# The fourth pair's weights asked for before the last token stores, and a pair's split in two

## The reference, cut to what matters

```python
# local attention: chunks of 32 queries, keys 16 left, 8 right, and 8 memory keys
out[:, :, c_start:c_end] = softmax(scale * q_c @ k_full.T) @ v_full

# Fourier mixing and first MLP
mixed = np.real(fft(fft(x, axis=1), axis=2))
u = x + mixed
un = (u - mu) / np.sqrt(var + 1e-06)
x = u + np.maximum(un @ w_ch1, 0.0) @ w_ch2          # 512 -> 2048 -> 512

# gated convolution
h = np.maximum(x @ w_in, 0.0)                        # 512 -> 1024
gate = 1.0 / (1.0 + np.exp(-conv3_over_tokens(h)))
y = (h * gate) @ w_out
```

## Time and profile before

| | us |
|---|---|
| median of three runs | 993.39 |
| lowest, highest | 991.74, 995.04 |
| profiled execution | 991.06 |
| its span in the trace | 989.3 |

### The profile page before, as it was taken

The page is one execution under the profiler, slowest core; times in us unless marked ns, Lnnn a source line. Parts: engine busy times, 40 slices in busy tenths (PEclk is TensorE's granted clock), DMA queues, the critical chain, the costliest instruction groups (busy, mean ns, idle before and its releaser), DMA issues.

```text
span 989.3 us, 15359 instructions
## 1 busy us (share of the span) xinstructions
PE 943.7 (95%) x6168; PEld 850.1 (86%) x6168; DVE 624.9 (63%) x1034; ACT 346.7 (35%) x583; POOL 221.1 (22%) x231
## 2 busy tenths in 40 slices
PE   5899997859999999999999999999999999999998
PEld 4788786858897998989989889898898898998997
DVE  5467759658586773776827767266486295393590
ACT  2444555314244231332312323124253254253341
POOL 5757758114020000000000000000024033042041
PEclk9999999889999999999999999999999999999999
DMA  9956733567435672544824536355120300301001
GB/s 336 356 178 235 277 120 108 217 230 283 184 142 231 215 260 67 195 147 155 308 79 161 181 117 233 129 160 179 60 70 1 128 1 22 106 0 42 22 1 64
DMA packets 50033, 148.41 MB, mean 150 GB/s; under 512 B 7856, under 2 KB 12080, under 8 KB 45616
## 3 DMA queue, kind: packets, MB, share of 16 engines
q1 hardware_dynamic: 44640, 85.16, 25.0%
q0 software_dynamic: 5184, 62.27, 16.8%
q10 hardware_dynamic: 144, 0.07, 0.0%
HBM read 115.50 MB, written 31.98 MB: 149 GB/s over the span
## 4 chain that ended last, share of the span: by engine, by line
PE 85%; DVE 5%; DMA 4%; POOL 3%; issue 1%; SPq 1%; ACT 1%; DVEq 0%; POOLq 0%; ACTq 0%
PE ps L995 25%; PE ps L975 22%; PE ps L1327 13%; PE ps L1337 13%; PE ps L543 5%; DMA k_win<-in_k 2%; PE ps L507 2%; DMA w_raw<-in_moe_w 1%; PE ps L1310 1%; PE ps L534 1%; PE ps L936 1%; DVE h_raw L890 1%; DVE w L813 1%; PE ps L517 1%; DVE h L894 1%
## 5 line engine op out<-in xcount | busy, mean ns | idle before, releaser
L995 PE MATMUL ps<-w,h 128*128 128x512 f32 x1152 | 267.3, 391 | 0.4 <-DVE h_raw L890 0.4
L995 PEld LDWEIGHTS ps<-w,h 128*128 128x128 f32 x1152 | 215.0, 188 | 44.6 <-DVE h_raw L890 0.8
L975 PE MATMUL ps<-x_hi,w 128*128 128x384 f32 x896 | 232.8, 338 | 11.5 <-DVE w L813 10.1
L975 PEld LDWEIGHTS ps<-x_hi,w 128*128 128x128 f32 x896 | 164.2, 190 | 12.8 <-DVE w L813 10.7
L890 DVE TENSOR_TENSOR h_raw<-h_raw,ps 128x384 f32<-128x384 f32 x224 | 122.8, 552 | 59.6 <-PE ps L975 53.5
L975 PE MATMUL ps<-x_lo,w 128*128 128x384 f32 x448 | 151.1, 337 | 0.0
L1327 PE MATMUL ps<-y_hi,v 128*128 128x384 f32 x512 | 130.6, 334 | 0.0
L806 ACT ACTIVATE h<-h_raw 128x384 fp32r<-128x384 f32 x128 | 67.0, 526 | 157.0 <-DVE h_raw L890 154.9
L1337 PE MATMUL ps<-v,g_hi 128*128 128x512 f32 x384 | 118.9, 391 | 0.0
L1395 POOL TENSOR_TENSOR g_lo<-conv,g_hi 128x768 fp32r<-128x768 f32 x32 | 68.8, 2154 | 185.7 <-ACT g_hi L1258 185.7
L1289 DVE SCALAR_TENSOR_TENSOR conv<-h_pad,taps,conv 128x768 f32<-128x768 f32 x64 | 100.5, 1570 | 2.3
(11 more groups left out here) (110 smaller groups left out, 1166.8 us busy)
## 6 DMA issues: line engine op xcount, KB each, us to landing
w<-w_scratch POOLq DMA_DIRECT2D x24, 1792.0 KB, 7.6
w_raw<-in_moe_w SPq DMA_DIRECT2D x80, 256.0 KB, 2.9
w_scratch<-w POOLq DMA_DIRECT2D x8, 1792.0 KB, 8.2
v_win<-in_v SPq DMA_DIRECT2D x48, 260.0 KB, 5.0
k_win<-in_k SPq DMA_DIRECT2D x48, 256.0 KB, 5.0
q_sb<-in_q SPq DMA_DIRECT2D x24, 256.0 KB, 4.6
y_scratch<-u SPq DMA_DIRECT2D x8, 768.0 KB, 4.6
y_in<-y_scratch SPq DMA_DIRECT2D x4, 1536.0 KB, 7.1
```

Of the source, the lines that this page charges most:

```text
L975: last = nc.tensor.matmul(result(n, i), a, b, start=(k == 0), stop=(k == 5))
L995: last = nc.tensor.matmul(ps[:, t, :], h[:, m, part, cols], w2[j % R2][:, weight], start=(m == 0 and i == 0), stop=(m == GROUP - 1 and i = ...
```

## The change

SP asks for pair 3's weights right after the stores of batch 2's tokens, ahead of the stores of batch 3's; that load no longer waits for the end of seq (only pair 2's does). POOL stores pair 0's weights ahead of the sums of pair 2, in mlp2. The tiles are renumbered so that the four sums and the three blocks each lie together, and a pair's split on ACT and DVE is two steps: `blocks1` on the three plain blocks (768 elements), which ACT does as soon as the load has landed, and `sums1` on the four sums (1024 elements) after POOL. DVE's `blocks1` also waits for the sums to be made. PE and the store wait for both. In `rest`, ACT does `blocks1` of pair n + 1 ahead of `keep_first(n)` and `sums1` behind it. `ORDER` has new places: in batch 3's end the new steps mlp14 to mlp16 (ACT) and mlp20 to mlp22 (DVE), `bl3.5` ahead of mlp10, `cm3.1` ahead of pair 2's split, which now stands among `mk3`; in batches 0 to 2 steps trade places with their neighbours; the tensor lines left out below are only wrapped anew. The core of the diff:

```diff
--- before.py
+++ after.py
...
-        "turn1.3 seq0.6 scores1.4 seq0.7 scores1.5 values1.1 dim0.1 turn1.4 values1.2 mix0.0 turn1.5 mix0.1 "
-        "values1.3 mix0.2 scores2.0 mix0.3 values1.4 mix0.4 mix0.5 scores2.1 turn2.0 values1.5 seq1.0 "
-        "scores2.2 seq1.1 turn2.1 seq1.2 turn2.2 seq1.3 scores2.3 seq1.4 values2.0 seq1.5 turn2.3 scores2.4 "
...
+        "turn1.3 seq0.6 scores1.4 seq0.7 values1.1 scores1.5 dim0.1 turn1.4 values1.2 mix0.0 turn1.5 mix0.1 "
+        "values1.3 mix0.2 scores2.0 mix0.3 values1.4 mix0.4 mix0.5 scores2.1 turn2.0 values1.5 seq1.0 turn2.1 "
+        "scores2.2 seq1.1 scores2.3 seq1.2 turn2.2 seq1.3 values2.0 seq1.4 turn2.3 seq1.5 scores2.4 values2.1 "
...
     "scalar": (
...
-        "split0.2 exp0.5 keep0.5 split0.3 exp1.0 bh0.0 split0.4 keep1.0 bh0.1 split0.5 bh0.2 exp1.1 bh0.3 "
-        "exp1.2 keep1.1 bh0.4 bh0.5 keep1.2 exp1.3 qs0.0 split1.0 bh0.6 mirror0.0 bh0.7 exp1.4 keep1.3 exp1.5 "
-        "qs0.1 keep1.4 mirror0.1 split1.1 keep1.5 split1.2 exp2.0 keep2.0 split1.3 exp2.1 bh1.0 split1.4 "
-        "bh1.1 keep2.1 exp2.2 bh1.2 split1.5 bh1.3 bh1.4 exp2.3 keep2.2 bh1.5 keep2.3 exp2.4 split2.0 qs1.0 "
+        "split0.2 exp0.5 keep0.5 split0.3 exp1.0 bh0.0 keep1.0 split0.4 bh0.1 split0.5 bh0.2 exp1.1 bh0.3 "
+        "exp1.2 keep1.1 bh0.4 bh0.5 keep1.2 exp1.3 qs0.0 split1.0 bh0.6 mirror0.0 bh0.7 exp1.4 keep1.3 qs0.1 "
+        "exp1.5 keep1.4 split1.1 mirror0.1 keep1.5 split1.2 exp2.0 split1.3 keep2.0 exp2.1 bh1.0 keep2.1 "
+        "split1.4 bh1.1 exp2.2 split1.5 bh1.2 exp2.3 bh1.3 keep2.2 bh1.4 bh1.5 split2.0 keep2.3 exp2.4 qs1.0 "
...
-        "qs2.1 split3.3 mirror2.1 split3.4 mlp1 bh3.0 split3.5 bh3.1 mlp2 mlp3 bh3.2 mlp7 bh3.3 bh3.4 mlp4 "
-        "bh3.5 mlp5 mlp8 mlp6 qs3.0 bh3.6 mirror3.0 bh3.7 mlp10 mlp9 qs3.1 mlp11 mirror3.1 mlp12 mlp13 "
+        "qs2.1 split3.3 mirror2.1 split3.4 mlp1 mlp14 bh3.0 split3.5 bh3.1 mlp2 mlp3 bh3.2 mlp7 bh3.3 bh3.4 "
+        "mlp4 bh3.5 mlp5 mlp15 mlp8 mlp6 qs3.0 bh3.6 mirror3.0 bh3.7 mlp16 mlp10 qs3.1 mlp9 mlp11 mirror3.1 "
+        "mlp12 mlp13 "
...
     "vector": (
...
-        "shift1.4 bl0.6 bl0.7 shift1.5 norm1.1 cm0.1 norm1.2 mk0.0 mk0.1 norm1.3 mk0.2 shift2.0 mk0.3 norm1.4 "
-        "mk0.4 shift2.1 mk0.5 norm1.5 bl1.0 shift2.2 bl1.1 mlp0 bl1.2 mlp1 bl1.3 shift2.3 mlp2 bl1.4 norm2.0 "
-        "bl1.5 shift2.4 norm2.1 cm1.0 bl1.6 shift2.5 bl1.7 norm2.2 shift3.0 cm1.1 norm2.3 mk1.0 mk1.1 norm2.4 "
-        "mk1.2 shift3.1 mk1.3 norm2.5 mk1.4 shift3.2 mk1.5 bl2.0 norm3.0 bl2.1 bl2.2 shift3.3 bl2.3 shift3.4 "
+        "shift1.4 bl0.6 bl0.7 norm1.1 shift1.5 cm0.1 norm1.2 mk0.0 mk0.1 norm1.3 mk0.2 shift2.0 norm1.4 mk0.3 "
+        "shift2.1 norm1.5 mk0.4 bl1.0 mk0.5 shift2.2 mlp0 bl1.1 shift2.3 bl1.2 mlp1 norm2.0 bl1.3 mlp2 bl1.4 "
+        "bl1.5 shift2.4 norm2.1 cm1.0 shift2.5 bl1.6 bl1.7 norm2.2 shift3.0 cm1.1 norm2.3 mk1.0 mk1.1 norm2.4 "
+        "mk1.2 shift3.1 mk1.3 norm2.5 mk1.4 shift3.2 mk1.5 norm3.0 bl2.0 bl2.1 bl2.2 shift3.3 bl2.3 shift3.4 "
...
-        "norm3.5 mk2.2 mk2.3 mlp6 mk2.4 mlp5 mk2.5 bl3.0 mlp9 bl3.1 mlp7 bl3.2 mlp8 bl3.3 mlp13 bl3.4 mlp10 "
-        "bl3.5 mlp11 mlp14 mlp12 cm3.0 bl3.6 bl3.7 mlp16 mlp15 cm3.1 mlp17 mk3.0 mk3.1 mk3.2 mk3.3 mlp18 "
-        "mk3.4 mlp19 mk3.5 "
+        "norm3.5 mk2.2 mk2.3 mlp6 mk2.4 mlp5 mk2.5 bl3.0 mlp9 bl3.1 mlp7 bl3.2 mlp8 bl3.3 mlp20 bl3.4 mlp13 "
+        "bl3.5 mlp11 mlp21 mlp10 cm3.0 mlp12 bl3.6 mlp14 bl3.7 mlp16 cm3.1 mlp17 mk3.0 mlp22 mk3.1 mlp15 "
+        "mk3.2 mk3.3 mlp18 mk3.4 mlp19 mk3.5 "
...
     "gpsimd": (
-        "tabs0.0 fold0.0 fold0.1 lower0.0 tabd0.0 fold0.2 lower0.1 fold0.3 lower0.2 fold0.4 lower0.3 fold0.5 "
-        "lower0.4 lower0.5 fold1.0 lower1.0 fold1.1 fold1.2 lower1.1 fold1.3 lower1.2 fold1.4 lower1.3 "
-        "fold1.5 lower1.4 lower1.5 fold2.0 fold2.1 lower2.0 lower2.1 fold2.2 fold2.3 lower2.2 fold2.4 "
+        "tabs0.0 fold0.0 fold0.1 lower0.0 tabd0.0 lower0.1 fold0.2 fold0.3 lower0.2 fold0.4 lower0.3 fold0.5 "
+        "lower0.4 lower0.5 fold1.0 lower1.0 fold1.1 lower1.1 fold1.2 fold1.3 lower1.2 fold1.4 lower1.3 "
+        "fold1.5 lower1.4 lower1.5 fold2.0 lower2.0 fold2.1 lower2.1 fold2.2 fold2.3 lower2.2 fold2.4 "
...
+            mlp_sync(sp, FOLDS)
             for i in range(FOLDS):
...
-    A11, S2, S1, S3, A12, S4, A22 = range(7)
+    S4, S3, S2, S1, A22, A11, A12 = range(7)
+    SUMS, BLOCKS = slice(S4, S1 + 1), slice(A22, A12 + 1)
...
-    w1_hi_ready, w1_ready = sem("w1_hi_ready"), sem("w1_ready")
+    a1_hi_ready, a1_ready, s1_hi_ready, s1_ready = (sem(f"{name}_ready") for name in ("a1_hi", "a1", "s1_hi", "s1"))
...
-        sp.dma_start(w1_raw[n % 3][:, A11:A12 + 1:A12 - A11, 1], w[2 * n][:, 0].rearrange("p (k c) -> p k c", k=2)
+        sp.dma_start(w1_raw[n % 3][:, A11:A12 + 1, 1], w[2 * n][:, 0].rearrange("p (k c) -> p k c", k=2)
...
-        sp.dma_start(w1_raw[n % 3][:, S1:A22 + 1:A22 - S1, 1], w[2 * n + 1][:, 0].rearrange("p (k c) -> p k c", k=2)
+        sp.dma_start(w1_raw[n % 3][:, S1:A22 + 1, 1], w[2 * n + 1][:, 0].rearrange("p (k c) -> p k c", k=2)
...
     def load_raw2(sp, j):
...
     def store_w1(pool, n):
-        pool.wait_ge(w1_ready, n + 1)
+        pool.wait_ge(a1_ready, n + 1)
+        pool.wait_ge(s1_ready, n + 1)
...
     def stream_w1(pool, n):
...
-        else:
+        elif i == 2:
...
     def on_scalar(act):
-        def weights1(n):
+        def blocks1(n):
+            act.wait_ge(ld_raw1[n % 3], 32 * (n // 3 + 1))
+            nc.scalar.activation(w1[n % 3][:, BLOCKS, 0], w1_raw[n % 3][:, BLOCKS, 1], ACT.Copy).then_inc(a1_hi_ready, 1)
...
+        def sums1(n):
...
-            nc.scalar.activation(w1[n % 3][:, :, 0], w1_raw[n % 3][:, :, 1], ACT.Copy).then_inc(w1_hi_ready, 1)
+            nc.scalar.activation(w1[n % 3][:, SUMS, 0], w1_raw[n % 3][:, SUMS, 1], ACT.Copy).then_inc(s1_hi_ready, 1)
...
         def weights2(j):
...
     def on_vector(dve):
-        def weights1(n):
-            dve.wait_ge(w1_hi_ready, n + 1)
-            nc.vector.tensor_tensor(w1[n % 3][:, :, 1], w1_raw[n % 3][:, :, 1], raw(w1[n % 3][:, :, 0]), ALU.subtract
-                                    ).then_inc(w1_ready, 1)
+        def lower1(n, part, ready):
+            nc.vector.tensor_tensor(w1[n % 3][:, part, 1], w1_raw[n % 3][:, part, 1], raw(w1[n % 3][:, part, 0]),
+                                    ALU.subtract).then_inc(ready, 1)
...
+        def blocks1(n):
...
+            dve.wait_ge(a1_hi_ready, n + 1)
+            dve.wait_ge(s_ready, n + 1)
+            lower1(n, BLOCKS, a1_ready)
...
+        def sums1(n):
+            dve.wait_ge(s1_hi_ready, n + 1)
+            lower1(n, SUMS, s1_ready)
...
         def weights2(j):
...
-        return (weights1, weights2, stats, variance, inverse_root, normalise, lower, lower_sums, combine, complete,
+        return (blocks1, sums1, weights2, stats, variance, inverse_root, normalise, lower, lower_sums, combine, complete,
...
     def on_tensor(pe):
...
-                pe.wait_ge(w1_ready, n + 1)
+                pe.wait_ge(a1_ready, n + 1)
+                pe.wait_ge(s1_ready, n + 1)
...
     def first_gpsimd(pool, k):
+        if k == 2:
+            store_w1(pool, 0)
...
     def first_scalar(act, k):
...
         elif k < 7:
...
         elif k < 10:
-            weights1(k - 7)
+            sums1(k - 7)
+        elif k > 13:
+            blocks1(k - 14)
...
     def first_vector(dve, k):
-        (weights1, weights2, stats, variance, inverse_root, normalise, lower, lower_sums, combine, complete,
+        (blocks1, sums1, weights2, stats, variance, inverse_root, normalise, lower, lower_sums, combine, complete,
...
         elif k < 16:
-            weights1(k - 13)
+            sums1(k - 13)
+        elif k > 19:
+            blocks1(k - 20)
...
-                    if n + 3 < PAIRS:
+                    if 0 < n < PAIRS - 3:
...
         def _(pool):
...
-            for n in range(PAIRS):
+            for n in range(1, PAIRS):
...
                 if n >= 2 and n + 1 < PAIRS:
...
         def _(act):
...
                     if n >= 2:
+                        early = 3 <= n + 1 < PAIRS and n + 1 not in (5, 6)
+                        if early:
+                            blocks1(n + 1)
...
-                        if 3 <= n + 1 < PAIRS and n + 1 not in (5, 6):
-                            weights1(n + 1)
+                        if early:
+                            sums1(n + 1)
...
                     if g == 0 and m in (0, 3):
-                        weights1(5 + m // 3)
+                        blocks1(5 + m // 3)
+                        sums1(5 + m // 3)
...
         def _(dve):
-            (weights1, weights2, stats, variance, inverse_root, normalise, lower, lower_sums, combine, complete,
+            (blocks1, sums1, weights2, stats, variance, inverse_root, normalise, lower, lower_sums, combine, complete,
...
                     if n >= 2:
+                        early = 3 <= n + 1 < PAIRS and n + 1 not in (5, 6)
...
```

(20 more changed lines are left out.)

## The result

| | before | changed |
|---|---|---|
| median of ten runs, us | 993.62 | 985.4 |
| lowest, highest | 991.74, 995.04 | 981.68, 990.54 |
| profiled execution | 991.06 | 982.31 |

The ratio is 0.9921, 95% interval 0.9901 to 0.9941: 7.8 us faster, 5.9 to 9.8 (the two medians differ by 8.2). The changed kernel's runs lie 9 us apart, those of before 3; on the chip of the first four experiments 24 runs of the kernel before lie 7.8 us apart (988.6 to 996.4), so a wide spread is not the changed kernel's alone.

What follows compares the result with a forecast made beforehand. PE, busy 95% of the span, was bounded by idle and half-clock stretches, chiefly 9.1 us waiting for pair 3's weights. Contraction 11.3 us earlier less 1.5 for the clock gave 9.8 us: 983.5 us forecast, range 979.0 to 988.5.

Steps and rivals of the forecast that it cites:

- L + 8.9: First contraction goes on 8.9 us after L, the landing of pair 4's load; L forecast 213.8, contraction 222.7.
- the 1.5 us that were to be paid for the clock: First contraction: PE idles 4.2 us, the clock then falls and costs 1.5 us of the gain.
- Part 1: Split in two, at dim3.0: starts at 169.5; an extra DVE instruction costs 0.3 us; mlp4 ends about 1.3 us earlier.
- Part 2: mix3.0 starts 3.5 us earlier after 1.2 us idle; full clock saves 1.5 us; pair 2 starts at 200.1.
- Part 3: Early load of pair 3: goes out at 187.3, lands by 194; pair 3 starts at 208.9, 12.9 us earlier.
- What is late next: After pair 3's start, pair 4's load gates the first contraction: 222.7, 11.3 us earlier, less 1.5 for the clock.
- Rival (2): Loads starve beside pair 3's store: gain only 5 to 6.5 us, time 987.5; chance 0.12.
- DVE against POOL: POOL's sums(4) beside DVE's additions with a PSUM operand take 3.2 us; otherwise 1.7 more and a gain of 8.1.
- Part 4: New order of the attention stage, batches 0 to 3: worth 0, ends -1 and +1 us.
- sign of being wrong: Among the listed signs: any new PE wait over 1 us ahead of 147 us.
- Rival (1): Pair 4's load lands in time and the clock holds: gain 12.9 to 13.8 us, time 980.3; chance 0.21.
- Rivals (3) to (5): Early load ineffective, 988.4 (0.07); pair 4's late load makes it slower, 997 (0.06); small losses eat the gain, 993 (0.05).

Runs made afterwards that it cites:

- the first four experiments: e1, e2, e3 and e4, each run beside the kernel before on one chip; ratios 0.9942, 1.0009, 1.0000 and 0.9874.
- e6: Changed kernel with POOL's sums of pair 4 ahead of pair 3's store; median 983.28 us, ratio 0.9898.
- e7: Changed kernel with pair 5's load ahead of pair 4's on SP; median 990.55 us, ratio 0.9971.
- e2: Kernel before with only the early load of pair 3 and early store of pair 0, no split, old order; median 994.11 us, ratio 1.0009.
- second repeat of the changed kernel: The changed kernel itself, unaltered, run and profiled again; median 984.76 us, ratio 0.9915 against the kernel before.
- e8: Kernel before with the new order of batch 3's end alone, no split, no early load; median 989.85 us, ratio 0.9956.
- e1: Changed kernel with pair 3's load put back behind the last token stores on SP; median 988.18 us, ratio 0.9942 against the kernel before.
- the repeats: The changed kernel itself, unaltered, run and profiled twice more; medians 983.7 and 984.76 us, ratios 0.9901 and 0.9915 against the kernel before.
- e5: e2's kernel with POOL's sums of pair 4 ahead of pair 3's store; median 989.19 us, ratio 0.9965 against the kernel before.
- e9: e4's kernel with POOL holding pair 3's sums until DVE's first addition that releases pair 2; median 979.43 us, ratio 0.9859 against the kernel before.
- e3: Kernel before with the new order of the attention stage alone; median 993.2 us, ratio 1.0000.
- e4: Changed kernel with pair 4's load ahead of the seven second-layer loads on SP; median 980.97 us, ratio 0.9874 against the kernel before.
- e4_again: The same kernel as e4, run again on e9's chip; median 980.19 us, ratio 0.9860 against the kernel before.

## Why the prediction was right, and where it was off

**The sum.** 9.8 us were forecast, 7.8 measured; 983.5 against 985.4, inside the range. The mechanism was that of the forecast: the early load moves what is late to pair 4's load, and L + 8.9 held to 0.1 us in five executions of the changed order (216.3, 218.9, 217.8, e6's 218.0 and e7's 223.1). That the number came so near is in part luck. The contraction came 8.8 us earlier and not 11.3, and the 1.5 us that were to be paid for the clock behind it were not paid in that execution; the two errors go against each other. And the profiled execution was the second quickest of the ten runs, 3.1 us under their median, where I had added 2.3.

**Part 1.** dim3.0 at 169.7, forecast 169.5, but after 2.85 us of idle and not 2.3; the execution was 0.3 us ahead already at mix2.0. Its 18 matmuls took 6.1 us and not 5.0 as before: the clock, which I had kept as it was and allowed 0.8 us for. mlp4 so ended at 188.8 and not at 187.2, no earlier than before (188.6). The change doesn't make this fall: e2, with the old order, took 6.2 us there, and the second repeat of the changed kernel 5.0.

The price of the split was wrong both ways. From pair 1 on it was too high. Both DVE instructions together take 2.08 us against 2.02 for one, so 0.06 and not 0.3. I had read the fixed part from L883's 1.28 us; DVE's subtraction for the four sums, the same 1024 elements, takes 1.21. The estimate of 0.16 us by the Trainium skill's formula (VectorE: DVE Perf Modes, the TRN2 errata) was nearer than mine. At pair 0, the one split that stands ahead of dim3.0, it was too low. There POOL makes sums beside it, and the three blocks took 1.48 us where pair 1's took 0.94:

```profile
166.04 1.48 DVE L820 TENSOR_TENSOR w<-w_raw,w 128x768 fp32r<-128x768 f32 x1
...
172.21 0.94 DVE L820 TENSOR_TENSOR w<-w_raw,w 128x768 fp32r<-128x768 f32 x1
```

With 1.28 us for pair 0's sums that is 2.76 us for the 2.01 of one instruction, and in all nine profiles with the split the blocks took 1.24 to 1.49 us there. The order alone (e8) left 2.54 us of idle before dim3.0, less than order and split together.

**Part 2.** The idle stretch before mix3.0 is 1.37 us, forecast 1.2, and the clock stayed full there; the 8.35 us became 1.53 + 5.23 = 6.8, forecast 6.8. With part 1 this was to bring pair 2 forward by 5.0 us, to 200.1. It started at 202.3, 2.9 us ahead of before, and at 202.2 in e1: 1.6 us are missing from part 1, 0.2 at mix3.0 and 0.4 before pair 2. That e1's runs were 5.8 us faster all the same doesn't bear out the 5.0, since its trace shows 2.8 of them. By e8 most of it is order.

**Part 3.** Pair 0's store had landed at 177.0, before it was needed, and the load went out at 188.8, 1.5 late by part 1 alone. Pair 3 started at 212.5, not 208.9: 1.6 from part 1, 0.4 from DVE beside POOL, and 1.6 from a fall of the clock in pair 2 that I hadn't forecast.

**What is late next** is the mis-sized term. L was 216.3, 2.5 later than forecast, all by the later request (210.3 for 207.1): the load took 5.96 us, forecast 6.7. DVE's own chain would have let the contraction go on 0.7 us earlier, so the gate held by little in that execution. The 1.5 us for a falling clock weren't paid there (3.1 us of idle; 1.6 us were paid in pair 2 instead); in the repeats (4.7 and 5.2 us of idle) 2.0 and 2.8 us were paid, in e6 (3.15 us) 1.6.

Rival (2), loads that starve beside the store, had 0.12. The early load brought pair 3's store forward by 9.1 us (212.9 for 222.05) and pair 4's second load by 4.0 (210.3 for 214.3). The distance from that load to that store was 2.6, 1.25 and 1.0 us in the three profiled executions of the changed kernel, where the load took 5.96, 6.25 and 7.29 us to land, and 0.8 and 0.0 us in e2 and e7, where it took 10.2 and 10.9. Only the last two stand out, and 7.29 perhaps: with no store beside it the load took 5.8 us in e5, 6.2 in e6 and 6.7 in the kernel before. Three of the ten runs (987.5, 989.2 and 990.5 us) had the time of rival (2) or more; no trace shows why. I should have seen that the load's worth depends on parts 1 and 2: without them the same load is worth nothing, and as a sum of parts (0 and 5.8) the change doesn't give its 7.8. My margins of rival (2) were taken from shares; 10.2 us for 256 KB with the store 0.8 us behind (e2) is the price itself.

**DVE against POOL.** Over sums(4) DVE had additions with a PSUM operand and the four sums took 3.2 us, as forecast. The Trainium skill, SBUF — State Buffer, SBUF: two separate sides, names as DVE instructions that share a lock with GpSimd those in a two-port mode and, against a GpSimd instruction that reads SBUF, those with two SBUF inputs. The trace agrees: beside those additions each sum took 0.74 us. But the same rule applied to sums(3), which I moved without asking what DVE does beside them: L911 has two SBUF inputs and took 0.99 us, and 0.55 in e9 with the sums held back. The slower split of pair 0 fits it as well.

**Part 4** and the rivals: e3 gives 0. One sign of being wrong did come, a wait over 1 us ahead of 147 us: 1.2 us for v_win. It cost nothing that shows (mix2.0 at 147.4, before 147.7), and e5's profile, with the old order, has one of 2.8. Rival (1) needed L by 212. Rivals (3) to (5) didn't come.

## What to carry to other kernels

When a load is asked for earlier, look for the next load of the same kind and for the next large store: the chain behind them is the same, and the store starts just when the work that you sped up ends. Measure parts together and alone; here two changes were worth 0 and 5.8 us and together 7.8 to 9.8, and putting pair 4's load first (e4) brought 3 to 6 us more. Profile the same kernel more than once before a difference of 2 us between two traces is read as the change: here the start of one and the same step (mix2.0) moved by 4 us and the clock fell now in one place, now in another. An idle stretch of 2 to 3 us can cost more than itself through the clock, but whether it does couldn't be told ahead from its length.

## What the runs showed of the hardware

A 256 KB load of SP's queue took 5.8 to 6.7 us behind seven others with no store beside it (e5, e6, before), and 10.2 us (e2) when POOL's 1.8 MB store was issued 0.8 us after it; behind nine others and with the store at once it took 10.9 (e7). With the store 1.0 to 2.6 us behind it took 6.0 to 7.3 us. DVE's subtraction of 768 elements took 1.24 to 1.49 us beside POOL's sums and 0.94 without them; its L911 0.99 and 0.55. The lower clock of PE came in some executions of the same instructions and not in others. After 1.88 us of idle before pair 2 it came in four of seven profiles, after 1.43 to 1.45 us there in none of seven. In the first contraction it came after 4.7 and 5.2 us of idle (the repeats), after 3.15 in e6 and 2.60 in e9, but not after 3.11 in the changed kernel's first profile, nor after 2.40 in e4 and e4_again.
